# Rests of every second weight piece by one GpSimd subtraction instead of two TensorE products and a ScalarE copy

## The reference

```python
for t in range(S):
    kt, vt, bt = (k_n[:, :, t], v[:, :, t], beta[:, :, t, None])
    y[:, :, t] = np.einsum('bhd,bhde->bhe', q[:, :, t], state)
    v_old = np.einsum('bhde,bhd->bhe', state, kt)
    state = state + bt[:, :, :, None] * np.einsum('bhd,bhe->bhde', kt, vt - v_old)
...
h = x @ w_in                      # (3072, 384) @ (384, 2048)
g = h * (1.0 / (1.0 + np.exp(-h)))
x = (g @ w_out)                   # (3072, 2048) @ (2048, 384)
...
do_compute = x @ w_skip > 0       # then top-1 of 8 experts, 384 -> 1024 -> 384
```

## Time and profile before

| | |
|---|---|
| median of 3 runs | 819.45 us (818.46 to 821.53) |
| profiled execution: time | 824.12 us |
| profiled execution: span in the trace | 822.3 us |
| mean granted TensorE clock | 0.989 of full speed |
| busy share of the span | TensorE 95%, VectorE 69%, ScalarE 44%, GpSimd 14% |

### The profile page before, as it was taken

One profiled execution on the slowest core, in us unless ns is written; L12 is line 12 of the kernel. 1 busy time (PEld: TensorE's weight loads), 2 busy tenths in 40 slices (PEclk: granted clock), 3 DMA queues, 4 the chain that ended last, 5 costly groups with the idle time before them and its releaser, 6 DMA issues.

```text
span 822.3 us, 28779 instructions
## 1 busy us (share of the span) xinstructions
PE 781.2 (95%) x12083; PEld 713.0 (87%) x12083; DVE 567.5 (69%) x1503; ACT 360.3 (44%) x1024; POOL 114.0 (14%) x287
## 2 busy tenths in 40 slices
PE   5877989999999999999999999999999999999993
PEld 3546878999989998899999999999999989999993
DVE  6969887877588775777867687654423577777751
ACT  3723433434435253453434535343443545656531
POOL 1000000001010010101002010010102153445542
PEclk9988999999999999999999999999999999999998
DMA  8772112121311223113130211211024447665610
GB/s 279 210 248 61 34 57 64 60 93 46 93 47 50 83 66 97 41 49 92 57 102 22 67 47 61 71 42 47 22 69 145 134 153 231 209 208 182 195 35 14
DMA packets 48094, 79.83 MB, mean 97 GB/s; under 512 B 5840, under 2 KB 35498, under 8 KB 47968
## 3 DMA queue, kind: packets, MB, share of 16 engines
q1 hardware_dynamic: 44544, 73.07, 27.7%
q0 software_dynamic: 3424, 4.93, 2.0%
HBM read 67.05 MB, written 13.19 MB: 98 GB/s over the span
## 4 chain that ended last, share of the span: by engine, by line
issue 73%; DMA 12%; POOL 8%; PE 3%; DVE 1%; POOLq 1%; ACT 0%; SPq 0%
DMA id_table<-token,slot 6%; DMA out<-kv_t,ids_all 5%; POOL idle L692 3%; PE psum L1003 2%; POOL id_table L737 2%; POOL out L773 1%; POOL kq_t L747 1%; DMA id_table<-x_sb 1%; POOL kq_t L799 1%; DMA x_sb<-kq 1%; PE psum L859 0%; PE psum L1004 0%; DMA ids_all<-id_table 0%; POOLq L769 0%; SPq L573 0%
## 5 line engine op out<-in xcount | busy, mean ns | idle before, releaser
L1037 PE MATMUL psum<-xt_hi,w_hi 128*128 128x256 f32 x768 | 225.1, 293 | 2.1 <-DVE xt_lo L1578 1.0
L1038 PE MATMUL psum<-xt_lo,w_hi 128*128 128x256 f32 x768 | 216.8, 282 | 0.0
L1039 PE MATMUL psum<-xt_hi,w_lo 128*128 128x256 f32 x768 | 216.6, 282 | 0.0
L1213 ACT ACTIVATE h_raw<-psum 128x256 f32<-128x256 f32 x192 | 73.7, 384 | 319.5 <-PE psum L1039 317.6
L1468 DVE TENSOR_TENSOR h_lo<-h_raw,h_hi 128x256 fp32r<-128x256 f32 x192 | 81.3, 423 | 156.5 <-ACT h_hi L1214 143.8
L1037 PEld LDWEIGHTS psum<-xt_hi,w_hi 128*128 128x128 f32 x768 | 144.5, 188 | 9.6 <-issue 2.2
L1039 PEld LDWEIGHTS psum<-xt_hi,w_lo 128*128 128x128 f32 x768 | 145.6, 190 | 0.0
L1038 PEld LDWEIGHTS psum<-xt_lo,w_hi 128*128 128x128 f32 x768 | 145.1, 189 | 0.0
L1061 PE MATMUL psum<-w_hi,h_hi 128*128 128x394 f32 x384 | 138.3, 360 | 0.8 <-DVE h_lo L1468 0.8
L1063 PE MATMUL psum<-w_hi,h_lo 128*128 128x394 f32 x384 | 131.2, 342 | 0.0
L1062 PE MATMUL psum<-w_lo,h_hi 128*128 128x394 f32 x384 | 131.0, 341 | 0.0
(11 more groups left out here) (187 smaller groups left out, 1094.6 us busy)
## 6 DMA issues: line engine op xcount, KB each, us to landing
kq_t<-kq SPq DMA_DIRECT2D x24, 512.0 KB, 3.5
bp<-moe_w SPq DMA_DIRECT2D x24, 512.0 KB, 5.3
kv_t<-kv SPq DMA_DIRECT2D x24, 384.0 KB, 3.2
bp<-moe_w SPq DMA_DIRECT2D x24, 384.0 KB, 4.6
kd<-kq SPq DMA_DIRECT2D x20, 256.0 KB
x_table<-x_sb SPq DMA_DIRECT2D x13, 392.0 KB, 3.0
out<-x_sb SPq DMA_DIRECT2D x12, 384.0 KB
bp<-moe_w_in SPq DMA_DIRECT2D x6, 512.0 KB, 6.3
```

Of the source, the lines that this page charges most:

```text
L1037: m(out, hi, x_hi, start=first, stop=False)
L1038: m(out, hi, x_lo, start=False, stop=False)
L1039: return m(out, lo, x_hi, start=False, stop=last)
L1213: a_.activation(h_raw[i % 2][:, :], up_ps[i % 2][:, 0:G2], ACT.Silu)
```

## The change

Pieces with an even number go the old way. For pieces with an odd number TensorE and ScalarE's second copy are left out; GpSimd holds for `w_half` and then subtracts `w_hi` from the staged piece, both in SBUF, into `w_lo`, and counts `w_pool`. What waited for a count of `w_rest` or `w_split` now waits for half of it, and in most places for `w_pool` too: loads of odd pieces, `load_rows`, `warm`, `rows`, the `mask` of step 1, the expert weights. `gram(1, 0)`, which only needs the PSUM banks, waits for `w_split` alone. The PSUM banks of the even pieces stay a pair that alternates.

```diff
             def load_weights(i):
-                after(sp, w_rest, i - NSTAGE + 1)
+                after(sp, w_pool if i % 2 else w_rest, (i - NSTAGE) // 2 + 1)
...
                 if k:
-                    sp.wait_ge(w_rest, (WP - 2, WP)[k - 1])
+                    for used in (w_rest, w_pool):
+                        sp.wait_ge(used, (WP // 2 - 1, WP // 2)[k - 1])
...
+            def weights(i):
+                if i % 2:
+                    _, width, _ = piece_of((w_in, w_out), (0, 1), i, PIECES, F, 0)
+                    hi, lo = chunks(w_hi, i), chunks(w_lo, i)
+                    hold(w_half, i + 1)
+                    g.tensor_tensor(lo, stage[i % NSTAGE][:, 0:width].rearrange("p (m n) -> p m n", n=hi.shape[2]), f32(hi), ALU.subtract).then_inc(w_pool, 1)
...
-            schedule(steps(turn=turn, place=place, first=first))
+            schedule(steps(weights=weights, turn=turn, place=place, first=first))
...
             def weights(i):
+                if i % 2:
+                    return
                 _, width, _ = piece_of((w_in, w_out), (0, 1), i, PIECES, F, 0)
                 pe.wait_ge(w_half, i + 1)
-                after(pe, w_split, i - 1)
+                after(pe, w_split, i // 2 - 1)
...
-                    bank = psum[:, 2 * (i % 2) + a, 0:half]
+                    bank = psum[:, i % 4 + a, 0:half]
...
                 cp(hi, stage[i % NSTAGE][:, 0:width].rearrange("p (m n) -> p m n", n=hi.shape[2])).then_inc(w_half, 1)
-                if i >= 1:
+                if i % 2:
                     rest_of(i - 1)
-                if i == WP - 1:
-                    rest_of(i)
...
                     if t == 1:
-                        dve.wait_ge(w_rest, WP)
+                        dve.wait_ge(w_rest, WP // 2)
+                        dve.wait_ge(w_pool, WP // 2)
                         dve.wait_ge(rows_used, KD)
```

More of the change, by code:

```diff
@@ L254, in program @@
         w_loaded = [sem(f"w_loaded{i}") for i in range(NSTAGE)]
-        w_half, w_rest, w_split = map(sem, ("w_half", "w_rest", "w_split"))
+        w_half, w_rest, w_split, w_pool = map(sem, ("w_half", "w_rest", "w_split", "w_pool"))
         xt_hi_ready, xt_lo_ready = map(sem, ("xt_hi_ready", "xt_lo_ready"))
@@ L659, in expert_weights @@
                     sp.dma_start(dst, src).then_inc(ew_loaded[n], 16)
-            sp.wait_ge(w_split, WP)
+            sp.wait_ge(w_split, WP // 2)
+            sp.wait_ge(w_pool, WP // 2)
             sp.wait_ge(pu_done, T)
@@ L871, in gram @@
                     if a == 0:
-                        pe.wait_ge(w_split, WP)
+                        pe.wait_ge(w_split, WP // 2)
                     else:
@@ L1007, in warm @@
             def warm(n, weights_done):
-                pe.wait_ge(w_split, weights_done)
+                pe.wait_ge(w_split, weights_done // 2)
+                pe.wait_ge(w_pool, weights_done // 2)
                 for _ in range(n):
@@ L1018, in rows @@
                     pe.wait_ge(route_in, 32)
-                    pe.wait_ge(w_split, WP)
+                    pe.wait_ge(w_split, WP // 2)
+                    pe.wait_ge(w_pool, WP // 2)
                 pe.wait_ge(rows_in[k], 16 * len(turned[k]))
@@ L1192, in rest_of @@
                 _, width, _ = piece_of((w_in, w_out), (0, 1), i, PIECES, F, 0)
-                act.wait_ge(w_rest, i + 1)
+                act.wait_ge(w_rest, i // 2 + 1)
                 lo = chunks(w_lo, i)
-                cp(lo, psum[:, 2 * (i % 2):2 * (i % 2) + 2, 0:width // 2].rearrange("p b (m n) -> p (b m) n", n=lo.shape[2])).then_inc(w_split, 1)
+                cp(lo, psum[:, i % 4:i % 4 + 2, 0:width // 2].rearrange("p b (m n) -> p (b m) n", n=lo.shape[2])).then_inc(w_split, 1)
             def weights(i):
@@ L1237, in split_scores @@
                     act.wait_ge(score_done, 1)
-                    act.wait_ge(w_split, WP)
+                    act.wait_ge(w_split, WP // 2)
+                    act.wait_ge(w_pool, WP // 2)
                     cp(scores(w_hi), score_ps).then_inc(score_hi, 1)
```

## The result

The changed kernel takes 827.13 us (median of 4 runs, 825.13 to 827.88), the kernel before 819.89 us on the same chip (4 runs, 818.46 to 821.53). The ratio is 1.0095, with a 95% interval of 1.0076 to 1.0115: by the ratio 7.8 us slower (the two medians lie 7.2 us apart). Its profiled execution took 825.13 us with a span of 823.2 us.

A forecast was written before the change was run, and what follows sets the result against it. A DMA was taken to set the scan's start, with VectorE 6.0 us from being the bound. Stops of 12.8 us on VectorE make `rest` 6.0 us later: 819.45 + 6.0 = 825.4 us, range 818.4 to 828.0 us.

The forecast's parts named there:

- What bounds the kernel: Opening: a DMA, the last third of transposed `w_out`, sets the scan's start; VectorE's chain is 6.0 us from being the bound.
- What is removed: Seven pieces on TensorE and seven ScalarE copies; VectorE's 1.91 us idle before the eviction goes, the last third lands 0.7 us earlier.
- The price of the subtraction: On GpSimd: 2.5 times the copy's slope, 2.32 us for 1024 columns and 1.78 for 768, plus a 0.17 us hold.
- What VectorE loses: Opening: each subtraction stops VectorE for its length; piece 1 costs 0, pieces 3 and 5 2.49 each, four others 7.80: 12.8 us.
- The constants: GpSimd's constants move behind piece 1: about two us of small writes, done before piece 3 comes, given no cost.
- Nothing behind gives time back: Behind `rest`: the rest of the program hangs on this chain, so the 6.0 us delay stays in full.
- TensorE's clock: First us of the scan: emptier TensorE may run at the lower clock, 1.2 GHz, adding 0 to 1.5 us.
- Not stopped: Rival: GpSimd doesn't stop VectorE, the DMA stays the bound, 818.8 us, no change; chance 0.16.
- loads close up: Rival: VectorE isn't stopped and loads close up, line 1024 ends 4.5 us earlier, 814.9 us; chance 0.03.
- cheap subtraction: Rival: VectorE is stopped, but at twice the copy's slope 823.2 us, at once the slope 819.5 us; chance 0.13.
- three accesses or more: Rival: the subtraction costs three accesses or more, delay 14.9 us, shift 8.1, 827.5 us; chance of over 827.5: 0.07.

The follow-up runs named there:

- the run with idle products: The changed kernel, with TensorE doing eight products that nobody reads for each odd piece: 825.60 us, ratio 1.0075 to the kernel before.
- constants first: The changed kernel with GpSimd's constants back ahead of piece 1: 827.27 us, ratio 1.0079 to the kernel before.
- the kernel without odd rests: The changed kernel without subtractions: GpSimd only holds and counts, and odd rests are zeros written once at the start: 820.34 us, ratio 0.9996 to the kernel before.
- the copy: The changed kernel with a GpSimd copy of the staged piece in place of each subtraction: 820.84 us, ratio 1.0008 to the kernel before.

## Why the prediction was right, and where its terms were off

**What bounds the kernel.** That VectorE was 6.0 us from being the bound was the step that failed in size. It was read from one execution, 4.7 us above the median, whose last third was late; another execution of the same kernel had 1.9 us. Against the median about 3.9 us were absorbed (stops of one execution less the shift of the time), where the prediction let 12.8 - 6.0 = 6.8 be absorbed. That the profiled execution stood high was noted there, but the same shift was put on the median; an execution that is late by a transfer has more slack than the median one.

**What is removed.** The 1.91 us before the eviction did go. The 0.7 us for the DMA side did not come: the last third ended at 58.97, against 57.20 + 1.94 = 59.14 before; the loads had stood still between 30 and 35 us. That was hidden either way.

**The price of the subtraction.** Predicted 2.32 and 1.78 us, measured 2.34 and 1.67.

**What VectorE loses.** Right in kind, in place and in direction: nothing at piece 1, six stops behind it. Predicted 12.8 us, measured 10.67. Of the 2.1 us between, 1.0 is the hold of 0.17 us, which the prediction added to each stop, 0.4 is the price of the smaller subtractions, and about 0.7 is what VectorE's own instruction had to do anyway. `turn_back` began at 62.19 (64.15 was predicted), `rest` at 67.92 (69.8).

**The constants.** "Done before piece 3 comes" was right and was no reason to put them at nothing: they stopped a `TENSOR_SCALAR` for 0.98 us. This term was missing. So was piece 1's own: the prediction has VectorE only reduce and transpose until 18.46, but two `TENSOR_SCALAR` stand at the end of that stretch. When VectorE comes early they are stopped too, for 2.9 us behind piece 1 and the constants in the run with idle products.

**Nothing behind gives time back.** Neither refuted nor shown. One pair of traces has 3.7 us less between `rest` and the end, another (constants first) 0.5 us, and the traces of all kernels differ there by 3.8 us.

**TensorE's clock.** It was given 0 to 1.5 us, in the first us of the scan. It was 0.50 at 65 to 75 us, but 0.50 at 65 to 70 in the kernel before's repeated run as well. New was the drop at 25 to 35 us. By the ratios, idle products took 1.6 us off the change and 2.1 us off the kernel without odd rests. In both cases the intervals overlap, and in the change the clock did not come back to 1.00. So the clock's share of the loss is not shown; the kernel without odd rests had the same low clock and no loss.

The sum: stops 1.15 us too large (12.8 against 11.65), absorption 2.9 too large, so 6.0 + 2.9 - 1.15 = 7.8 us. Two errors of opposite sign brought the forecast near, and that is luck.

**The rivals.** *Not stopped* and *loads close up* fell with the first timeline. The *cheap subtraction* fell with 2.34 us; the copy shows what it would have given. The time came within 0.4 us of the 827.5 of *three accesses or more*, but the price was not that rival's.

The Trainium skill, SBUF — State Buffer, section Who interferes with whom, was cited for a lock that holds for the whole instruction. The traces agree in the direction that was open: 0.16 us became 2.44.

## What to carry to other kernels

GpSimd isn't free beside a VectorE that is busy with two-input instructions on SBUF: count each GpSimd subtraction or copy there as a stop of VectorE for its whole length, and look whether VectorE's chain has that much slack in several executions, not in one. What moves to GpSimd goes beside VectorE's transposes and reductions, or where VectorE waits. Before an engine is relieved, run the kernel with the work left out: here that showed no gain that can be measured (0.9996), and 0.3% with TensorE kept at work (0.9970).

## What the runs showed of the hardware beyond that

- Which VectorE instructions stop depends on both sides. GpSimd's subtractions stopped two-input instructions and `TENSOR_SCALAR` in SBUF, its copies two-input instructions (0.16 to 1.11 us); its memsets stopped only `TENSOR_SCALAR` (0.13 to 1.71 and 0.18 to 1.94 us) and left 0.41 us lanes at 0.41. A transpose of 128x1024 (1.97 us, against 1.92 to 2.01 with GpSimd idle) and a reduction (1.22 us either way) ran beside a subtraction unharmed.
- Small instructions in a row hold as one: the train of constants kept a 0.13 us instruction for 1.11 us, and two subtractions in a row kept one for 4.82 us. Not always: at one of the six later pairs a lane instruction of 1.79 us ended between the two, and the next lasted 1.64.
- GpSimd took 2.34 us for a subtraction of 1024 columns, 1.03 for a copy and 0.94 for a memset.
